# Attention stage: unsplit softmax weights for key tiles 0, 2 and 4, low parts on VectorE, a new order of slots and of the sync queue

## The reference, cut to what matters

```python
# 16 heads (2 x 8), 768 positions, 64 columns
mask = q_bucket[:, :, :, None] == k_bucket[:, :, None, :]    # 6 sign bits of q @ proj, k @ proj
scores = np.where(mask, scale * (q @ k.T), -1e9)
attn = np.exp(scores - max(scores)); attn /= attn.sum(-1) + 1e-9
x = (attn @ v).transpose(0, 2, 1, 3).reshape(B, S, 512)
x = (sigmoid(causal_conv5(x)) * (x @ w_val)) @ w_out
u = x + real(fft2(x)); un = layernorm(u)
out = u + relu(un @ w_ch1) @ w_ch2
```

## Time and profile before

| | us |
|---|---|
| median of 3 runs (783.83 to 794.24) | 784.6 |
| profiled execution | 781.99 |
| its span, first to last instruction | 780.1 |
| first weighing of V to the last | 50.9 to 375.6 |

### The profile page before, as it was taken

How to read it: one execution, slowest core, us unless ns; L and a number is a source line. 1 busy time by engine, 2 the same in 40 slices (tenths; PEclk the granted TensorE clock), 3 DMA queues, 4 the chain that set the end, 5 groups by cost and what they waited for, 6 DMA issues and landing times.

```text
span 780.1 us, 10303 instructions
## 1 busy us (share of the span) xinstructions
PE 701.6 (90%) x3696; PEld 647.9 (83%) x3696; DVE 418.7 (54%) x573; ACT 278.4 (36%) x424; POOL 381.9 (49%) x283
## 2 busy tenths in 40 slices
PE   2588889788888879878999999999999999999998
PEld 1388888787878778877989899998999999999897
DVE  3365578778888787797485467942122221212112
ACT  2146564455465454565352444211111111111110
POOL 1047778767878787788286697488100000000000
PEclk9589999999999999997999999999999999999999
DMA  9443645544544635111012112323010000001001
GB/s 246 116 123 98 155 118 139 129 113 107 144 113 112 158 106 129 50 31 42 17 50 61 41 42 75 88 85 95 11 40 0 0 28 13 0 0 41 1 0 41
DMA packets 33608, 57.67 MB, mean 74 GB/s; under 512 B 9232, under 2 KB 15632, under 8 KB 33568
## 3 DMA queue, kind: packets, MB, share of 16 engines
q1 hardware_dynamic: 33568, 57.14, 27.8%
HBM read 31.81 MB, written 3.24 MB: 45 GB/s over the span
## 4 chain that ended last, share of the span: by engine, by line
PE 71%; DVE 17%; DMA 4%; SPq 2%; issue 2%; POOL 2%; ACT 0%; DVEq 0%; POOLq 0%
PE psum L1057 63%; DVE max_col L808 4%; DVE neg_parts L818 2%; DMA a2k<-hash_bits 2%; DVE gate L862 1%; DVE qk_lo L794 1%; POOL p_lo L524 1%; DMA flag_dram<-a2q 1%; PE psum L1133 1%; DVE neg_rest L820 1%; PE psum L1138 1%; PE psum L1139 1%; PE psum L1135 1%; PE psum L1136 1%; DVE gate L859 1%
## 5 line engine op out<-in xcount | busy, mean ns | idle before, releaser
L524 POOL TENSOR_TENSOR p_lo<-probs,p_hi 128x768 fp32r<-128x768 f32 x96 | 190.2, 1996 | 66.4 <-ACT probs L647 65.1
L1028 DVE SCALAR_TENSOR_TENSOR h_lo<-psum,h_hi 128x384 fp32r<-128x384 f32 x64 | 35.7, 558 | 182.7 <-ACT h_hi L769 182.7
L808 DVE TENSOR_REDUCE max_col<-psum 128x1 f32<-128x768 f32 x96 | 91.6, 954 | 76.7 <-PE psum L1057 76.1
L644 ACT ACTIVATE p_hi<-psum 128x768 fp32r<-128x768 f32 x96 | 78.0, 813 | 104.6 <-PE psum L1057 103.0
L769 ACT ACTIVATE h_hi<-psum 128x384 fp32r<-128x384 f32 x64 | 31.5, 492 | 214.5 <-PE psum L1057 214.5
L1057 PE MATMUL psum<-a1k,a1q 128*128 128x384 f32 x192 | 74.2, 386 | 26.8 <-DMA a2k<-hash_bits 17.8
L1057 PE MATMUL psum<-unt_hi,w_hi 128*128 (+1 forms) x256 | 86.9, 339 | 0.0
L1057 PE MATMUL psum<-unt_lo,w_hi 128*128 (+1 forms) x256 | 86.3, 337 | 0.0
L1057 PE MATMUL psum<-unt_hi,w_lo 128*128 (+1 forms) x256 | 85.9, 336 | 0.0
L647 ACT ACTIVATE probs<-psum 128x768 f32<-128x768 f32 x96 | 77.3, 805 | 0.0
L1057 PE MATMUL psum<-w_lo,h_hi 128*128 128x512 f32 x192 | 75.9, 395 | 0.0
(11 more groups left out here) (124 smaller groups left out, 1561.6 us busy)
## 6 DMA issues: line engine op xcount, KB each, us to landing
stg_w<-in_w SPq DMA_DIRECT2D x32, 256.0 KB, 2.6
qk_raw<-in_qk SPq DMA_DIRECT2D x16, 384.0 KB, 5.1
...
```

Of the source, the lines that this page charges most:

```text
L524: pool.tensor_tensor(p_lo[i % PBUF][:, :], probs[i % PBUF][:, :], bits(p_hi[i % PHBUF][:, 0:S]), ALU.subtract).then_inc(p_lo_ready, 1)
L644: act.activation(halves(p_hi[i % PHBUF][:, 0:S]), ring[ring_st(i) % 2], ACT.Exp, scale=SCALE).then_inc(p_hi_ready, 1)
L808: dve.tensor_reduce(max_col[:, i % T:i % T + 1], s_ps, AX.XY, ALU.max).then_inc(max_done, 1)
L1028: dve.scalar_tensor_tensor(h_lo[:, half], psum[:, j % 2, 0:HALF], 0.0, bits(h_hi[:, half]), ALU.max, ALU.subtract).then_inc(h_lo_ready, 1)
```

## The change

- Only key tiles 1, 3 and 5 (`SPLIT`) still have `p_hi`, `p_lo`, `vh` and `vl`; for them `weigh_v` is six matmuls as before. For tiles 0, 2 and 4 ScalarE makes only `probs` (float32, with the column of ones), and `weigh_v` is two matmuls of plain float32, `v1` x `probs`.
- V is loaded straight into `v1` (float32, the other half of its columns preset to one); `hi_v` and `lo_v` work on the three split tiles.
- `lo_probs`, now 48 of them, moves from GpSimd to VectorE, ahead of the slot's maximum.
- `S_LEAD` goes from 10 to 11, `max_parts` one slot and the hash one slot forward; `reciprocals` and the convolution one and four slots back, `scale_x` and the return of the reciprocals later.
- The sync queue has a new order: flag and reciprocals are stored and spread in separate steps, `stack_bits` follows the odd head's `stack` directly, `load_qk` comes later, `load_wa` one slot later, while the `split_weights` that frees its buffer moves from a head's second slot to its sixth, behind `lo_v`.

```diff
-ST_LEAD, S_LEAD = 2, 10
-FIRST = -20
+ST_LEAD, S_LEAD = 2, 11
+FIRST = -21
+SPLIT = (1, 3, 5)
...
             def load_v(n):
...
-                    sp.wait_ge(vh_ready, n - 1)
                     sp.wait_ge(vl_ready, n - 1)
-                sp.dma_start(v_raw[n % 2][:, :], v[n // H, n % H, :, :].rearrange("(p t) d -> p (t d)", t=T)).then_inc(v_loaded[n % 2], 16)
+                    sp.wait_ge(pv_done, T * (n - 1))
+                sp.dma_start(tiles(v1[par][:, :])[:, :, par * D:(par + 1) * D],
+                             v[n // H, n % H, :, :].rearrange("(p t) d -> p t d", t=T)).then_inc(v_loaded[par], 16)
...
-            for g in range(FIRST, UNITS + T):
+            for g in range(FIRST, UNITS + 2 * T + 3):
                 pair, n = g // (2 * T), g // T
-                if g % (2 * T) == 10 and 0 <= pair + 3 < NPAIR and pair + 3 >= RAWS // 2:
-                    load_qk(2 * (pair + 3))
-                    load_qk(2 * (pair + 3) + 1)
+                if g % T == 1 and 1 <= n <= NH:
+                    fold_den(n - 1)
+                    if n + 1 < NH:
+                        load_v(n + 1)
+                if g % T == 4 and 1 <= n <= NH:
+                    store_rec(n - 1)
+                if g % T == 0 and 2 <= n <= NH + 1:
+                    spread_rec(n - 2)
                 if g % (2 * T) == 6 and 0 <= pair + 2 < NPAIR:
                     stack(2 * (pair + 2))
                 if g % (2 * T) == 10 and 0 <= pair + 2 < NPAIR:
                     stack(2 * (pair + 2) + 1)
-                if g % (2 * T) == 0 and 0 <= pair + 1 < NPAIR:
-                    stack_bits(pair + 1)
-                if g % T == 2:
-                    if 2 <= n + 2 < NH:
-                        load_v(n + 2)
-                        load_wa(n + 2)
-                    if 1 <= n <= NH:
-                        spread_rec(n - 1)
-                if g % T == 4 and 0 <= n + 1 < NH:
-                    spread_flag(n + 1)
-                if g % T == 1 and 1 <= n <= NH:
-                    fold_den(n - 1)
+                if g % (2 * T) == 11 and 0 <= pair + 2 < NPAIR:
+                    stack_bits(pair + 2)
+                if g % T == 5 and 0 <= n + 1 < NH:
+                    store_flag(n + 1)
+                if g % T == 1 and 0 <= n < NH:
+                    spread_flag(n)
+                if g % (2 * T) == 2 and 2 <= pair + 2 < NPAIR:
+                    load_qk(2 * (pair + 2))
+                    load_qk(2 * (pair + 2) + 1)
+                if g % T == 3 and 2 <= n + 2 < NH:
+                    load_wa(n + 2)
...
@@ gpsimd, slots
-                if 0 <= g + 1 < UNITS:
-                    lo_probs(g + 1)
-                if g % T == 3 and 0 <= n + 1 < NH:
+                if g % T == 4 and 0 <= n + 1 < NH:
                     lo_v(n + 1)
-                if g % T == 1 and 0 <= n < NH:
+                if g % T == 5 and 0 <= n < NH:
                     split_weights(n)
-                if g % T == 4 and 1 <= n <= NH:
-                    scale_x(n - 1)
-                    pool.wait_ge(x_ready, n)
+                if g % T == 2 and 2 <= n <= NH + 1:
+                    scale_x(n - 2)
+                    pool.wait_ge(x_ready, n - 1)
@@ scalar, exps
-                act.activation(halves(p_hi[i % PHBUF][:, 0:S]), ring[ring_st(i) % 2], ACT.Exp, scale=SCALE).then_inc(p_hi_ready, 1)
+                if is_split(i):
+                    k = splits_until(i)
+                    if k >= PHBUF:
+                        act.wait_ge(pv_done, split_unit(k - PHBUF) + 1)
+                    act.activation(halves(p_hi[k % PHBUF][:, 0:S]), ring[ring_st(i) % 2], ACT.Exp, scale=SCALE).then_inc(p_hi_ready, 1)
@@ scalar, slots
-                if g % T == 2 and 0 <= n + 1 < NH:
+                if g % T == 3 and 0 <= n + 1 < NH:
                     hi_v(n + 1)
@@ vector, slots
+                if 0 <= g + 1 < UNITS and is_split(g + 1):
+                    lo_probs(g + 1)
                 if 0 <= g + S_LEAD < UNITS:
                     maximum(g + S_LEAD)
-                if g % T == 1 and 0 <= n + 1 < NH:
+                if g % T == 0 and 0 <= n + 1 < NH:
                     max_parts(n + 1)
...
-                slot, tap = (g - 18) // (2 * T), (g - 18) % (2 * T) // 2
-                if 0 <= slot < NPAIR - 1 and (g - 18) % 2 == 0 and tap < KCONV:
+                slot, tap = (g - 22) // (2 * T), (g - 22) % (2 * T) // 2
+                if 0 <= slot and (g - 22) % 2 == 0 and tap < KCONV:
                     convolve(slot, tap)
@@ tensor, weigh_v
+                if not is_split(i):
+                    pe.wait_ge(probs_ready, i + 1)
+                    pe.matmul(first, v1[par][:, w], probs[i % PBUF][:, 0:HALF], start=start, stop=stop)
+                    pe.matmul(last, v1[par][:, w], probs[i % PBUF][:, HALF:PCOLS], start=start, stop=stop).then_inc(pv_done, 1)
+                    return
```

More of the change, by code:

```diff
@@ L40, with splits_until, is_split, split_unit @@
 UNITS = T * NH
-ST_LEAD, S_LEAD = 2, 10
-FIRST = -20
+ST_LEAD, S_LEAD = 2, 11
+FIRST = -21
+SPLIT = (1, 3, 5)
+def splits_until(i):
+    return i // T * len(SPLIT) + sum(j < i % T for j in SPLIT)
+def is_split(i):
+    return i % T in SPLIT
+def split_unit(k):
+    return k // len(SPLIT) * T + SPLIT[k % len(SPLIT)]
 def turn_slot(n):
@@ L49, in hash_slot @@
 def hash_slot(pair):
-    return 2 * T * pair - 14
+    return 2 * T * pair - 15
 def turns_until(g):
@@ L109 @@
 CREDIT = 1
-CONSTS = 1 + 2 * PHBUF + 4
+CONSTS = 1 + 2 * PHBUF + 2 * PBUF + 2
 X_SLOTS = (80, 82, 84, 86)
@@ L285, in build @@
         max_rows = sem("max_rows")
-        flag_stored = sem("flag_stored")
+        flag_stored = [sem(f"flag_stored{i}") for i in range(2)]
         flag_loaded = [sem(f"flag_loaded{i}") for i in range(2)]
@@ L490, in _ @@
                 pool.memset(bits(p_hi[i][:, S + 1:PCOLS]), 0.0).then_inc(consts_ready, 1)
+            for i in range(PBUF):
+                pool.memset(probs[i][:, S:S + 1], 1.0).then_inc(consts_ready, 1)
+                pool.memset(probs[i][:, S + 1:PCOLS], 0.0).then_inc(consts_ready, 1)
             for par in range(2):
-                own, rest = (slice(D, P), slice(0, D)) if par else (slice(0, D), slice(D, P))
-                pool.memset(bits(tiles(vh[par][:, :])[:, :, rest]), 1.0).then_inc(consts_ready, 1)
-                pool.memset(bits(tiles(vl[par][:, :])[:, :, rest]), 0.0).then_inc(consts_ready, 1)
+                rest = slice(0, D) if par else slice(D, P)
+                pool.memset(tiles(v1[par][:, :])[:, :, rest], 1.0).then_inc(consts_ready, 1)
             pool.wait_ge(consts_ready, CONSTS)
@@ L513, in lo_v @@
                 par = n % 2
-                own = slice(par * D, (par + 1) * D)
                 pool.wait_ge(vh_ready, n + 1)
@@ L808, in maximum, with lo_probs @@
                 dve.tensor_reduce(max_col[:, i % T:i % T + 1], s_ps, AX.XY, ALU.max).then_inc(max_done, 1)
+            def lo_probs(i):
+                k = splits_until(i)
+                dve.wait_ge(probs_ready, i + 1)
+                dve.tensor_tensor(p_lo[i % PBUF][:, 0:S], probs[i % PBUF][:, 0:S], bits(p_hi[k % PHBUF][:, 0:S]), ALU.subtract).then_inc(p_lo_ready, 1)
             def max_parts(n):
@@ L987, in lo_un @@
                 dve.tensor_tensor(part(unt_lo), tile(psum[:, 6 + t % 2, :]), bits(part(unt_hi)), ALU.subtract).then_inc(unt_lo_ready, 1)
-            for tap in range(3, KCONV):
-                convolve(NPAIR - 2, tap)
+            reciprocals(NH - 1)
             dve.wait_ge(x_ready, NH - 1)
             gate_values(0, 0)
-            reciprocals(NH - 1)
             gate_values(0, 1)
@@ L997, in _ @@
                 lo_x(1, c)
+            for tap in range(1, KCONV):
+                convolve(NPAIR - 2, tap)
             for tap in range(KCONV):
@@ L1131, in weigh_v @@
                         pe.wait_ge(sums_ready, n)
-                pe.wait_ge(p_hi_ready, i + 1)
-                pe.matmul(first, vh[par][:, w], hi[:, 0:HALF], start=j == 0, stop=False)
-                pe.matmul(last, vh[par][:, w], hi[:, HALF:PCOLS], start=j == 0, stop=False)
+                if not is_split(i):
[3 more added lines that the diff above has]
+                    return
@@ L1135, in weigh_v @@
+                k = splits_until(i)
+                hi, lo = p_hi[k % PHBUF], p_lo[i % PBUF]
+                w = slice(k % len(SPLIT) * P, (k % len(SPLIT) + 1) * P)
+                pe.wait_ge(p_hi_ready, k + 1)
+                pe.matmul(first, vh[par][:, w], hi[:, 0:HALF], start=start, stop=False)
+                pe.matmul(last, vh[par][:, w], hi[:, HALF:PCOLS], start=start, stop=False)
                 pe.matmul(first, vl[par][:, w], hi[:, 0:HALF], start=False, stop=False)
-                pe.matmul(last, vl[par][:, w], hi[:, HALF:PCOLS], start=False, stop=j == T - 1)
@@ L1137, in weigh_v @@
-                pe.wait_ge(p_lo_ready, i + 1)
-                pe.matmul(first, vh[par][:, w], lo[:, 0:HALF], start=False, stop=j == T - 1)
```

(7 more changed lines are left out.)

79 lines of the change are left out of this document (42 added, 37 removed).

## The result

The changed kernel takes 739.9 us (median of four runs, 739.7 to 740.5) against 784.2: a ratio of 0.945, 95% interval 0.943 to 0.946. The forecast was 763 with a range of 742 to 786.

What follows compares the result with a forecast made beforehand. In the 324.7 us stage of weighing V no engine is full; TensorE loses 48.9 us in waits and some 20 us to a lower clock. The terms sum to -19.6: 782.0 to 762.4, forecast 763, range 742 to 786.

Steps and rivals of the forecast that it cites:

- plain f32: Weighing of V, even key tiles: two plain float32 matmuls for six, 0.70 us each, +17 us over 48 units.
- GpSimd's low parts: TensorE's waits for the low parts that GpSimd makes: they go, -3.5 us.
- neg_parts: TensorE's waits for the six small operations on the maxima: all go, -25.5 us.
- max_col: TensorE's waits for the maximum, VectorE now making 48 low parts: 10 us in place of 1.9, +8.
- sums and what stands with them: Waits for sums before a head's first weighing: 1 us stays of 7.3, -6.3.
- hash bits: Bit DMAs behind load_wa in the sync queue: scores 2.4 us late in six pairs, 14.4 against 10.7, +3.7.
- clock: TensorE's granted clock in the stage: loss falls from 20 us to 7, -13.
- the stretch ahead of the stage: One more unit before the first weighing costs 2.7 us, one less in the stage saves 0.7: +2.
- A: Rival: the hash bits are in time, load_wa needing to be free only 2.4 us earlier; 742 us, chance 0.17.
- B: Rival: VectorE is the bound if its meetings with GpSimd stay as they are; about 784 us, chance 0.18.
- C: Rival: plain float32 weighing matmuls are cheap, as the transposes; 721 us, chance 0.05.
- D: Rival, slower side: plain float32 weighing matmuls are dear; 841 us with weight loads not hidden, chance 0.06.

Runs made afterwards that it cites:

- broadcast_ahead: The changed kernel with a 384 KB transfer of the flag row into an unread spare tile put right ahead of the hash bits: 764.2 us, ratio 0.973.
- wa_free: The changed kernel with each weight chunk loaded (load_wa) in slot 0 of the head before it needs it, not the fourth slot: 739.6 us, ratio 0.942.
- pool_lo_even: wa_free_pool_lo with key tiles 0, 2 and 4 split instead of 1, 3 and 5: 758.5 us, ratio 0.968.
- wa_free_pool_lo: wa_free with the 48 low parts made by GpSimd instead of VectorE, still tiles 1, 3 and 5 split: 737.5 us, ratio 0.941.
- pool_busy: wa_free with 96 subtractions on GpSimd that nobody needs, one a unit, on a spare tile: 773.6 us, ratio 0.985.
- all_split_pool: The changed kernel with all six tiles split, all low parts on GpSimd, and the weight load of wa_free: 799.0 us, ratio 1.018.

## Why the prediction was right in direction and short in size

Put side by side for the stage, forecast and measured: plain f32 +17, +11.5; GpSimd's low parts -3.5, -3.5; neg_parts -25.5, -25.5; max_col +8, +2.1; sums and what stands with them -6.3, -5.5 (1.8 us are left); hash bits +3.7, -6.0; clock -13, -20.2; the stretch ahead of the stage +2, +3.8. The measured ones sum to -43.3, and the profiled times differ by 42.1 (782.0 to 739.9): they tell 1.2 us too much, and leave nothing for the 2 us that I gave to fewer gaps. Four terms hold the error, all on one side: bits 9.7, clock 7.2, max_col 5.9, plain f32 5.5.

*The hash bits (the step that failed).* I had them land 4.6 us behind their issue "with a little for the six 192 KB DMAs in front", for h + 12.2 against due h + 9.8, so 2.4 late. The issue came as forecast: h, the end of the hash, was 195.42, load_wa was released at 197.27 (h + 1.85, forecast h + 2.2) and the second bit transfer issued at h + 7.4 (forecast h + 7). The due time, 206.04 less the wait of 0.61, was h + 10.0. But the scores went 3.2 us behind that issue, not 4.6. The 4.6 was read from a row in which the flag's spread, 384 KB, stood right ahead in the queue, and the change takes just that away. I named it and gave it no weight, and took 0.6 more for the stack's own DMAs. broadcast_ahead puts such a transfer back: 3.9 to 5.0 us behind the issue, which also came 0.2 to 0.9 later than in the changed kernel. So the waits were 0.6 to 1.2 us and not 2.4. The block at load_wa itself was forecast (some 10 us a head: 119.8 in 14), and in time it cost nothing that wa_free can show.

*The clock.* I let four of six late bits bring a dip. With the waits at a third of their forecast length, they brought none. This term leans on the one before it, so I had counted one misreading twice: 9.7 us of waits, and most of the 7.2 of clock (1.9 of these are that the kernel before lost 21.9 us and not the 20 I took).

*Plain f32.* Four passes was close as a price, 0.645 us against 4 x 0.176 = 0.70; the term was mis-sized by 5.5 us. The Trainium skill (FP8 and Floating Point Precision, TensorE Precision Notes) counts four passes. The trace's time is 8% below that and does not show the passes themselves.

*VectorE's lateness.* 4.0 us of waits for max_col, not 10. The queue in slot 6 was the right place: 3.7 of the 4.0 us stand behind it. It made the scores 0.53 to 0.55 us late in three pairs, where I had 0.7 in every one, and once, where the tap met GpSimd (2.59 us in place of 1.01), 2.1, where I had half a microsecond for meetings in every pair. That one wait also brought the only dip of the clock, 1.7 us. The low parts' own time was right (0.95 median for q and k, 1.11 in the mean here).

*Right, but by half a reason.* The 25.5 us for neg_parts went as forecast, and with GpSimd out of the way the six short operations take 0.17 to 0.18 us, as the undisturbed one in the earlier trace rows. I had given two reasons, one slot more of cover and GpSimd mostly idle, and did not tell them apart. pool_lo_even does in part: its short operations are slow and yet nothing waits for neg_parts, so the added slot seems to be enough for that wait; what the slow operations then cost shows as 20.3 us for max_col. And I saw VectorE making the low parts as part of freeing GpSimd. wa_free_pool_lo gets the same with 48 of them on GpSimd, and pool_lo_even loses it with the same 48 one slot over. What counts is where GpSimd's instructions stand, above all that none begins in the slot of the short operations, and less, beside the taps. In the change as made, VectorE's part brings nothing that can be measured: it spends 52 us of VectorE to free GpSimd, which was free where it mattered.

*The rivals.* A (742, bits in time) came nearest: the bits were nearly in time. But not by its reason, that load_wa "only has to be free 2.4 us earlier": load_wa came free as forecast, and the landing was shorter. That the number fits within 2 us is partly luck, since 4.7 us of waits for the bits remained, and plain f32 and max_col were some 11 us cheaper than in its sum. B needed the meetings to stay as they were, and they didn't; pool_busy comes nearest to that world, at 774. C and D fell with the price of plain f32: the transposes of the earlier trace rows, 0.27 us for as many columns, were no guide to it.

Still open: why all_split_pool is 14 us slower than the kernel before, what the added slot of cover is worth by itself, and whether the old order with half the tiles split would do as well; the last two were not tried.
